# Queries and keys split ahead of their transposes, and a second score pass on exchanged query halves

## What is computed

```python
B, H, S, D = 4, 8, 576, 64
scores = matmul(q, k.T) / 8.0
s_pos = maximum(s, 0.0); cum = cumsum(s_pos, -1)
bias = -(cum[:, :, :, None] - cum[:, :, None, :])
scores = where(causal, -1e9, scores + minimum(bias, 0.0))
attn = exp(scores - max(scores)); attn = attn / (sum(attn) + 1e-09)
x = matmul(attn, v)                       # 32 heads of 576 x 64
# then: layer norm + relu MLP (512 -> 2048 -> 512), a rank-32 mix over tokens, a second MLP
```

## Time and profile before

| | |
|---|---|
| time, median of 3 runs (lowest, highest) | 1116.39 us (1112.28, 1117.29) |
| the profiled execution | 1115.07 us, its span 1113.3 us |
| granted TensorE clock, mean | 0.992 |
| busy share of the span | TensorE 94%, its weight load 84%, VectorE 73%, ScalarE 50%, GpSimd 31% |
| instructions | 21040 |
| DMA | 118.71 MB in 156260 packets, mean 107 GB/s |

### The profile page before, as it was taken

The page is one execution under the profiler, slowest core; times in us unless marked ns, Lnnn a source line. Parts: engine busy times, 40 slices in busy tenths (PEclk is TensorE's granted clock), DMA queues, the critical chain, the costliest instruction groups (busy, mean ns, idle before and its releaser), DMA issues.

```text
span 1113.3 us, 21040 instructions
## 1 busy us (share of the span) xinstructions
PE 1051.2 (94%) x6936; PEld 931.8 (84%) x6936; DVE 811.7 (73%) x1732; ACT 557.2 (50%) x1265; POOL 339.6 (31%) x377
## 2 busy tenths in 40 slices
PE   6788888888797999999999999999999999999998
PEld 5677777777687898889888889888889888888887
DVE  6899999999558768767767757976865866765532
ACT  5788888888444344444444434443423432433321
POOL 1154453211116433333324232333232423332100
PEclk9999999999898999999999999999999999999999
DMA  5745545445241321322231343432142133223131
GB/s 155 233 120 132 126 120 130 127 119 159 83 134 64 108 76 57 123 68 77 76 114 58 114 151 107 156 112 82 62 138 96 66 100 121 75 84 114 58 127 44
DMA packets 156260, 118.71 MB, mean 107 GB/s; under 512 B 86496, under 2 KB 131552, under 8 KB 156192
## 3 DMA queue, kind: packets, MB, share of 16 engines
q1 hardware_dynamic: 156192, 117.80, 35.2%
HBM read 98.82 MB, written 18.95 MB: 106 GB/s over the span
## 4 chain that ended last, share of the span: by engine, by line
PE 89%; DVE 3%; ACT 3%; issue 2%; DMA 1%; SPq 1%; POOL 0%; ACTq 0%; DVEq 0%; POOLq 0%
PE ps_up L751 9%; PE ps_up L752 9%; PE ps_up L753 9%; PE ps_acc L798 6%; PE ps_acc L797 6%; PE ps_acc L799 6%; PE ps_s L798 5%; PE ps_s L797 5%; PE ps_s L799 5%; PE ps_x L681 5%; PE ps_s L651 3%; PE ps_pt L662 3%; ACT prob L928 2%; PE ps_up L662 2%; PE ps_up L627 2%
## 5 line engine op out<-in xcount | busy, mean ns | idle before, releaser
L751 PE MATMUL ps_up<-z,w 128*128 128x256 f32 x896 | 255.6, 285 | 4.7 <-DVE z L1270 3.8
L752 PE MATMUL ps_up<-z,w 128*128 128x256 f32 x896 | 254.4, 284 | 0.0
L753 PE MATMUL ps_up<-z,w 128*128 128x256 f32 x896 | 254.4, 284 | 0.0
L564 POOL TENSOR_TENSOR w_f<-raw 128x256 f32<-128x256 f32 x64 | 69.0, 1078 | 412.1 <-DMA raw<-in_moe_w_ch 397.4
L751 PEld LDWEIGHTS ps_up<-z,w 128*128 128x128 f32 x896 | 172.3, 192 | 10.6 <-DVE z L1270 4.2
L752 PEld LDWEIGHTS ps_up<-z,w 128*128 128x128 f32 x896 | 172.5, 193 | 5.1
L753 PEld LDWEIGHTS ps_up<-z,w 128*128 128x128 f32 x896 | 172.8, 193 | 0.0
L797 PE MATMUL ps_acc<-w_hi,h 128*128 128x512 f32 x320 | 126.7, 396 | 1.9 <-DVE x_res L1296 1.9
L798 PE MATMUL ps_acc<-w_lo,h 128*128 128x512 f32 x320 | 126.8, 396 | 0.0
L799 PE MATMUL ps_acc<-w_hi,h 128*128 128x512 f32 x320 | 126.2, 394 | 0.0
L1093 ACT ACTIVATE h<-cs 128x768 fp32r<-128x768 f32 x64 | 54.1, 846 | 126.8 <-DVE cs L1383 126.8
(11 more groups left out here) (170 smaller groups left out, 2642.7 us busy)
## 6 DMA issues: line engine op xcount, KB each, us to landing
raw<-in_moe_w_ch SPq DMA_DIRECT2D x80, 512.0 KB, 3.6
ncum_b<-ncum_dram SPq DMA_DIRECT2D x32, 288.0 KB, 3.5
x_in<-x_dram SPq DMA_DIRECT2D x18, 512.0 KB, 4.3
k_raw<-in_k SPq DMA_DIRECT2D x64, 128.0 KB, 2.5
u_dram<-x_in SPq DMA_DIRECT2D x9, 512.0 KB, 2.8
q_raw<-in_q SPq DMA_DIRECT2D x32, 128.0 KB, 3.2
v_raw<-in_v SPq DMA_DIRECT2D x32, 128.0 KB, 2.2
w_f<-in_moe_w_ch SPq DMA_DIRECT2D x4, 1024.0 KB, 8.1
```

Source lines behind the costliest of these rows:

```text
L564: pool.tensor_tensor(to[:, I5, 1], a21, a22, ALU.add).then_inc(s1_done, 1)
L751: nc.tensor.matmul(bank, w_hi, z_hi, start=(start and c == 0), stop=False, skip_group_check=True)
L752: nc.tensor.matmul(bank, w_hi, z_lo, start=False, stop=False, skip_group_check=True)
L753: last = nc.tensor.matmul(bank, w_lo, z_hi, start=False, stop=(stop and c == 1), skip_group_check=True)
```

## The change

- Queries, keys and their last tile are no longer split after the transposes but before. GpSimd makes the high and low part of the raw rows side by side (`split_rows`: `split_queries`, `split_keys`, `split_last`, two instructions each), for head u+2 ahead of `split_values(u)`. TensorE then transposes 128-column tiles that hold both, so that high parts come out in partitions 0 to 63 and low parts in 64 to 127.
- ScalarE copies the queries out of PSUM with one instruction (`copy_q`, where `q_high` was), VectorE the keys (`copy_k`, where `k_low` was) and the last tile of both (`copy_last`). `q_low`, `k_high` and `last_high` are gone.
- The two score passes use the same keys (hi over lo). The first has the queries as they are (hi with hi, lo with lo), the second has the query halves exchanged, in `q_swap`. The exchange is made by DMA inside SBUF, two transfers of 64 partitions for the 512 columns and two for the last 64: `swap_queries`, `swap_last`.
- Keys are loaded once, in the row order of the queries; the last tiles are loaded once. `load_last` runs one head further ahead.
- SP's list has a new order. Buffers of raw rows are free when GpSimd has split them, not when TensorE has transposed them.
- The slices of w2 are split in halves (high or low part), spread over heads 2 to 29.
- TensorE's score tile 0 waits for the exchanged queries too, tile 4 for the exchanged last tile.

```diff
             def load_q(u):
-                wait(sp, qt_done, u)
+                wait(sp, q_lo_done, u)
                 sp.dma_start(q_raw[:], flat_rows(q_f, u)).then_inc(q_loaded, 16)
             def load_k(u):
-                wait(sp, kt_done, u)
-                for a in range(2):
-                    sp.dma_start(k_raw[:, :, a], whole_tiles(k_f, u)).then_inc(k_loaded, 16)
+                wait(sp, k_lo_done, u)
+                sp.dma_start(k_raw[:], flat_rows(k_f, u)).then_inc(k_loaded, 16)
             def load_last(u):
-                waits_apart(sp, (lt_done, u))
+                waits_apart(sp, (l_lo_done, u))
                 for flat, to in ((q_f, slice(0, LAST)), (k_f, slice(LAST, P))):
-                    sp.dma_start(last_raw[to], last_tile(flat, u).unsqueeze(1).to_broadcast([LAST, 2, D])).then_inc(last_loaded, 16)
+                    sp.dma_start(last_raw[to, 0], last_tile(flat, u)).then_inc(last_loaded, 16)
+            def swap_queries(u, p):
+                waits_apart(sp, (q_done, u + 1))
+                for to, of in ((slice(0, D), slice(D, P)), (slice(D, P), slice(0, D))):
+                    sp.dma_start(q_swap[p][to, 0:FULL].bitcast(F32), qk[p][of, 0, 0:FULL].bitcast(F32)).then_inc(q_swapped[p], 16)
+            def swap_last(u, p):
+                waits_apart(sp, (l_done, u + 1))
+                for to, of in ((slice(0, D), slice(D, P)), (slice(D, P), slice(0, D))):
+                    sp.dma_start(q_swap[p][to, FULL:S].bitcast(F32), qk[p][of, 0, FULL:S].bitcast(F32)).then_inc(l_swapped[p], 16)
             def head_alone(m, p, first=False):
                 u = 2 * m + p
+                if exists(u + 3):
+                    load_q(u + 3)
+                    load_k(u + 3)
+                if exists(u + 1):
+                    swap_last(u + 1, 1 - p)
+                if exists(u + 3):
+                    load_last(u + 3)
                 if exists(u + 2):
-                    load_last(u + 2)
+                    load_sums(u + 2, p)
+                    swap_queries(u + 2, p)
                 if exists(u + 1):
                     load_v(u + 1)
-                if exists(u + 2):
-                    load_sums(u + 2, p)
-                if exists(u + 3):
-                    load_q(u + 3)
                 if not first:
                     store_head(*before(m, p))
-                if exists(u + 3):
-                    load_k(u + 3)
...
             load_last(1)
             load_q(2)
             load_k(2)
+            for p in range(2):
+                swap_queries(p, p)
+            swap_last(0, 0)
+            load_last(2)
...
+            def split_rows(u, x, split, loaded, transposed, hi_done, lo_done):
+                pool.wait_ge(*loaded)
+                waits_apart(pool, (transposed, u))
+                pool.tensor_tensor(split[:, :, 0, :], x[:], one[:].unsqueeze(2).to_broadcast(x.shape), ALU.mult).then_inc(hi_done, 1)
+                pool.wait_ge(hi_done, u + 1)
+                pool.tensor_tensor(split[:, :, 1, :], x[:], split[:, :, 0, :].bitcast(F32), ALU.subtract).then_inc(lo_done, 1)
...
+            split_queries(0)
+            split_keys(0)
+            split_last(0)
+            split_queries(1)
+            split_keys(1)
+            split_last(1)
             pool.wait_ge(pads_done, 1)
             for u in range(HEADS):
+                if u + 2 < HEADS:
+                    split_queries(u + 2)
+                    split_keys(u + 2)
+                    split_last(u + 2)
                 split_values(u)
-                if 4 <= u < 4 + JC:
-                    split_second(u - 4)
+                for half in range(halves(u), halves(u + 1)):
+                    split_second(half // 2, half % 2)
...
+            def transpose_rows(bank, split):
+                to = bank.rearrange("d (n t) -> d t n", t=QT - 1)
+                for t in range(QT - 1):
+                    last = nc.tensor.transpose(to[:, t], twice(split[:, t]).bitcast(F32), ident)
+                return last
...
             def scores(m, p, i):
                 u = 2 * m + p
-                q2, k_hi, k_lo = (a[p] for a in (q2s, k_his, k_los))
                 if i == 0:
-                    pe.wait_ge(q_lo_done, u + 1)
-                    pe.wait_ge(k_lo_done, u + 1)
-                    pe.wait_ge(l_lo_done, u + 1)
+                    pe.wait_ge(q_done, u + 1)
+                    pe.wait_ge(k_done, u + 1)
+                    pe.wait_ge(l_done, u + 1)
+                    pe.wait_ge(q_swapped[p], 32 * (m + 1))
+                if i == QT - 1:
+                    pe.wait_ge(l_swapped[p], 32 * (m + 1))
...
-                    for n, kk in enumerate((k_hi, k_lo)):
-                        last = nc.tensor.matmul(bank, q2[:, i * P:(i + 1) * P], kk[:, lo:hi], start=(n == 0), stop=(n == 1 and not diag))
+                    for n, qq in enumerate((qk[p][:, 0], q_swap[p][:])):
+                        last = nc.tensor.matmul(bank, qq[:, i * P:(i + 1) * P], qk[p][:, 1, lo:hi], start=(n == 0), stop=(n == 1 and not diag))
...
+            def copy_q(m, p):
                 act.wait_ge(qt_done, 2 * m + p + 1)
+                nc.scalar.activation(qk[p][:, 0, 0:FULL], up[0][:, 0:FULL], ACT.Copy, scale=-SCALE).then_inc(q_done, 1)
...
+            def copy_k(m, p):
+                dve.wait_ge(kt_done, 2 * m + p + 1)
+                nc.vector.tensor_copy(qk[p][:, 1, 0:FULL], k_bank(2 * m + p)[:, 0:FULL]).then_inc(k_done, 1)
+            def copy_last(m, p):
+                dve.wait_ge(lt_done, 2 * m + p + 1)
+                nc.vector.tensor_tensor(qk[p][:, :, FULL:S], up[0][:, 0:P].rearrange("p (a n) -> p a n", a=2),
+                                        last_scale[:].unsqueeze(2).to_broadcast([P, 2, LAST]), ALU.mult).then_inc(l_done, 1)
```

More of the change, by code:

```diff
@@ L161, in chain_kernel @@
             prob_2_0 = sbuf("prob_2_0", [P, FULL], F32, small)
-            q2s = [sbuf(f"q2{p}", [P, SP_PAD], F32R, small) for p in range(2)]
+            q_swap = [sbuf(f"q_swap{p}", [P, SP_PAD], F32R, small) for p in range(2)]
             prob_3 = sbuf("prob_3", [P, FULL], F32, small)
@@ L234, in chain_kernel @@
         l_hi_done, l_lo_done = sem("l_hi_done"), sem("l_lo_done")
+        q_done, k_done, l_done = sem("q_done"), sem("k_done"), sem("l_done")
+        q_swapped, l_swapped = [sem(f"q_swapped{p}") for p in range(2)], [sem(f"l_swapped{p}") for p in range(2)]
         v_hi_done, v_split = sem("v_hi_done"), sem("v_split")
@@ L615, in transpose_q @@
-                for t in range(QT - 1):
-                    last = nc.tensor.transpose(bank[:, t], q_raw[:, t], ident)
-                last.then_inc(qt_done, 1)
+                waits_apart(pe, (q_lo_done, u + 1), (l_done, u))
+                transpose_rows(up[0], q_split).then_inc(qt_done, 1)
             def transpose_k(m, p):
                 u = 2 * m + p
-                pe.wait_ge(k_loaded, 32 * u + 32)
+                pe.wait_ge(k_lo_done, u + 1)
                 if not (isinstance(u, int) and u == 0):
-                    pe.wait_ge(q_lo_done, u + 1)
@@ L625, in transpose_k @@
[L625 to L628, removed]
+                    pe.wait_ge(q_done, u + 1)
+                transpose_rows(k_bank(u), k_split).then_inc(kt_done, 1)
             def transpose_last(m, p):
                 u = 2 * m + p
-                pe.wait_ge(last_loaded, 32 * u + 32)
-                pe.wait_ge(k_lo_done, u + 1)
@@ L635, in transpose_last @@
-                nc.tensor.transpose(up[0][:, 0:P], twice(last_raw[:]), ident).then_inc(lt_done, 1)
+                pe.wait_ge(l_lo_done, u + 1)
+                pe.wait_ge(k_done, u + 1)
+                if isinstance(u, int) and u == 0:
+                    pe.wait_ge(q_done, u + 1)
+                nc.tensor.transpose(up[0][:, 0:P], twice(last_split[:, 0]).bitcast(F32), ident).then_inc(lt_done, 1)
             def scores(m, p, i):
                 u = 2 * m + p
-                q2, k_hi, k_lo = (a[p] for a in (q2s, k_his, k_los))
@@ L948, in head_alone @@
                 probs_high(m, p, 1)
-                if not final:
-                    last_high(*after(m, p))
                 exponential(m, p, 3)
@@ L955, in head_alone @@
                 if more:
-                    q_high(*second(m, p))
+                    copy_q(*second(m, p))
                 if final:
@@ L966, in head_alone @@
                 probs_high(m, p, 4)
-                if more:
-                    k_high(*second(m, p))
                 if not final:
@@ L1064, in prepare @@
                     second_high(j)
-            q_high(0, 0)
-            k_high(0, 0)
-            last_high(0, 0)
+            copy_q(0, 0)
             exponential(0, 0, 0)
-            q_high(0, 1)
+            copy_q(0, 1)
             exponential(0, 0, 1)
-            k_high(0, 1)
             attention(act, head_alone)
@@ L1201, in head_alone @@
                     weights_low(0)
-                if more:
-                    q_low(*second(m, p))
                 if not final:
```

(2 more changed lines are left out.)

76 lines of the change are left out of this document (32 added, 44 removed).

## The result

The changed kernel takes 1140.14 us (median of 4 runs, 1138.43 to 1141.77); the kernel before, run beside it, 1115.73 us (1112.28 to 1117.29). The ratio is 1.020, 95% interval 1.017 to 1.023: about 24 us slower, clearly more than nothing. The direction that was held likeliest is right, the size is not, and 1140 lies above the range of 1113 to 1138.

What follows compares the result with a forecast made beforehand. Bound: a loop of TensorE's queue and ScalarE's tile-3 copy and tile-4 exponential, 8.28 us a head. Sum: 1115.1 + 5.0 (start) - 1.5 (w2 loads) + 1.7 (TensorE) + 4 (SP's queue) = 1124.3, say 1124 us; range 1113 to 1138.

Steps and rivals of the forecast that it cites:

- What bounds a head: Attention stage: a loop of TensorE's queue (6.75 us) and ScalarE (1.53 us), 8.28 us, without VectorE.
- Rival D: Attention heads: the freed VectorE and ScalarE shorten the head, TensorE's wait goes at most whole; 1089 us, chance 0.08.
- SP's queue: SP's issuing of transfers in the looped heads: a little over the loop's period, +4 us.
- 6.7 + 4s: SP's time per head in us after the change, with four swaps at s each; 8.66 us forecast.
- s: Price of issuing one swap on SP: taken as 0.49 us, between 0.34 and 0.66.
- Rival C: SP's queue: swaps as dear to issue as the doubled last tile, 0.66 us; 1142 us, chance 0.10.
- The lead of 3 us: Looped heads: some 3 us that SP can fall behind before its lateness costs time.
- The start: First heads: splits and swaps queued behind load_k(2) delay the first score to 14.6 us; +5.0 us, bounds +4.3 and +6.4.
- The w2 loads: Early heads: TensorE's waits for last-tile loads behind 2 MB of weights go; -1.5 us, bounds -2.6 and 0.
- TensorE, +1.7: Query transposes in the loop, as wide as the keys': 287 ns each, not 273; +1.7 us for 30 heads.
- Rival E: Key transposes, written to PSUM with a stride of four columns, slow down; 1137 us, chance 0.05.
- GpSimd: Splits of raw rows on GpSimd: 0.58 + 0.69 us for 256 columns, 6.9 of 8.33 us a head; costs 0 in steady state.

Runs made afterwards that it cites:

- x1: The changed kernel without its four swap transfers per head and the waits on them, cross products of high and low parts left out; 1112.32 us, ratio 0.996.
- x5: x1 with the exponential of tile 4 issued on ScalarE ahead of copy_q and the tile-3 copy; 1099.96 us, ratio 0.985.
- x2: The kernel before with four unread transfers inside SBUF, of 64 partitions each, added per looped head on SP; 1172.27 us, ratio 1.050.
- x10: The kernel before with two unread transfers inside SBUF, of 128 partitions each, added per looped head on SP; 1139.77 us, ratio 1.019.
- x3: The changed kernel with the first query swap and first last-tile swap moved earlier in SP's list; 1135.76 us, ratio 1.017.
- x6: The changed kernel, complete, with the two loads of v per head issued by ScalarE and not by SP; 1125.12 us, ratio 1.007.
- x8: The changed kernel without the two last-tile swaps per head, cross products of that tile left out; 1119.61 us, ratio 1.002.
- x11: The kernel before with two unread transfers of 128 partitions from DRAM into SBUF added per looped head on SP; 1129.83 us, ratio 1.012.

## Why the prediction was off

**What bounds a head: right.** The loop of TensorE and ScalarE, with no VectorE in it, was read from the earlier trace rows. x1 takes 0.7 to 1.0 us a head off both engines and keeps the 8.28 us. Rival D is out. It has a condition that I had not seen: with ScalarE's order changed the same relief gives 12 us (x5).

**SP's queue: the right mechanism, the wrong size, and this is the step that failed.** The formula 6.7 + 4s holds: with the 0.57 us measured it gives 8.98, and SP took 9.01. I took s = 0.49, the row of a 64-row load from DRAM, because it had the same number of partitions, and wrote that the price was in no row. For these transfers within SBUF partitions hardly set it (x2 and x10: 0.59 and 0.56), and the same transfer costs less out of DRAM (0.56 against 0.42). A nearer row stood in the trace of before, and I had overlooked it: the store of a head's last 64 rows, which has the same number of partitions and its source in SBUF.

```profile
101.35 0.58 SPq L385 DMA_DIRECT2D x_dram<-x_head  x1
```

SBUF as the source is not the whole price either: the store of the other 512 rows, out of 128 partitions, takes 0.42. The choice between 0.49 and the doubled tile's 0.66 decided over some 18 us. At 0.57, and with TensorE's period as it was measured, my reckoning gives 26 x (8.98 - 8.34) - 3 = 13.6 us for the loop, where I had put 4 and 1.7; 15.5 were lost. The term is steep: 0.01 us of s is worth 1 us of time. With such a slope a point value and half of C in the range were too little.

This step is the largest part of the miss and not all of it. The profiled execution, 1141.8 us, lies 17.5 above the forecast of 1124.3: 9.8 in the loop, 4.4 at the w2 loads, 1.5 in the last head, 1.3 in the rest of the span, 0.5 at the start. With s at 0.57 and the other terms as forecast the sum would have been 1132, still inside the range. Rival C, with a chance of 0.10, decides from 0.55 on, so the case is C's; that its 1142 lies so near the 1140 measured is luck, for it stands for s = 0.66.

**The lead of 3 us: not shown.** After the stalls of the w2 loads, TensorE next stands as long as this for a swap at 89.74, four heads later, when SP at the measured pace had lost 4 x 0.67 = 2.7 us:

```profile
89.74 0.32 PE L711 MATMUL ps_s<-qk 128*128 128x128 f32 x1 [1.05 <-DMA q_swap<-qk]
```

That fits a lead of about 3 us, but how far ahead SP was after those stalls no row tells, so it is not shown.

**The start: right.** The first score was put at 14.6 us, the total at +5.0 (+4.3 to +6.4); 15.05 and +5.5 were measured. The mechanism is the one named, the swaps behind `load_k(2)`: they were issued at 12.01, and x3, which moves them, gets 3.9 us back.

```profile
15.05 0.45 PE L711 MATMUL ps_s<-qk 128*128 128x128 f32 x1 [5.35 <-DMA q_swap<-qk]
```

**The w2 loads: wrong in sign.** I let both waits for raw rows go and kept 1 us for `swap_last(3)`. They did go, but two swaps of the last tile wait in their place, the first of which I had not reckoned:

```profile
40.87 0.40 PE L711 MATMUL ps_acc<-qk 128*128 128x288 f32 x1 [1.15 <-DMA q_swap<-qk]
...
52.04 0.41 PE L711 MATMUL ps_acc<-qk 128*128 128x288 f32 x1 [2.61 <-DMA q_swap<-qk]
```

3.76 us against 2.58. A load has its slack of a head or more; a swap is made between a copy and its use and has little, so it is the worse thing to queue behind 2 MB. The other 1.6 us of this stretch is the second head, 9.84 us long against 8.27, which runs while the clock is below full (0.85 as a mean from 20 to 30 us). It is not the swaps' doing: x1 has none, and its second head takes 9.83 us (clock 0.83 as a mean from 20 to 30 us).

**TensorE, +1.7: 0.** The query transposes stayed at 273 ns, although twice the partitions go in. The difference to the keys in the earlier trace rows was not one of width; what it is no run shows. **Rival E** is refuted: 286 ns with the stride.

**GpSimd: right.** Its splits, with those of the kernel after from 100 to 250 us beside VectorE's copy of the keys:

```profile
L579 POOL TENSOR_TENSOR q_split<-q_raw,q_split 128x256 fp32r<-128x256 f32 x17 | 12.4, 731 | 1.3
...
L1164 DVE CAST qk<-ps_up 128x512 fp32r<-128x512 f32 x17 | 11.7, 686 | 0.0
...
L577 POOL TENSOR_TENSOR q_split<-q_raw,one 128x256 fp32r<-128x256 f32 x17 | 10.4, 612 | 0.0
```

0.61 + 0.73 against the predicted 0.58 + 0.69, and nobody waits for GpSimd in the loop.

**What I had not reckoned with: the clock.** TensorE's wait of 1.05 us at 89.74 costs more than itself. Behind it, after only 1.4 us of work, comes the wait for the exponential that every head has:

```profile
92.22 0.77 PE L722 MATMUL ps_pt<-ident_f,prob 64*128 64x64 f32 x5 [1.08 <-ACT prob L979]
```

By itself this second wait doesn't lower the clock: before, it comes in every head while the granted clock is 1.00. Here the clock falls just ahead of 92 us. The windows (stretch, length, busy time and instructions of TensorE, its weight load, VectorE, ScalarE and GpSimd, granted clock, DMA share, GB/s):

```profile
90.00:92.00 2.00, 1.14 (x12) 0.83 (x11) 0.94 (x4) 1.27 (x4) 1.64 (x3) 0.95 0.46 140
92.00:94.00 2.00, 1.78 (x10) 1.69 (x11) 0.94 (x3) 0.90 (x4) 1.92 (x3) 0.50 0.12 24
94.00:96.00 2.00, 2.00 (x11) 1.60 (x9) 1.18 (x4) 0.60 (x2) 1.62 (x3) 0.50 0.78 193
96.00:98.00 2.00, 2.00 (x11) 1.48 (x10) 1.26 (x5) 1.26 (x4) 0.00 (x0) 0.50 0.84 206
...
100.00:103.00 3.00, 2.30 (x23) 1.99 (x21) 1.80 (x7) 2.53 (x5) 2.45 (x3) 1.00 0.28 78
```

For 6 us the granted clock is 0.50, that is 1.2 GHz. The head that holds the swap wait takes 9.59 us, the one behind it, over half of it at half the clock, 11.16. From 60 to 260 us the mean granted clock is 0.97 after the change, 0.96 in x10, 0.88 in x2, and 1.00 before and in x1, x6 and x8. In the loop I read it as a symptom more than a cause: while TensorE is slow SP gains on it, the next heads run at 8.28 to 8.58 again, and the mean is back near SP's pace (8.91 and 9.01). SP's own rounds show no trace of it: from 62 us on, up to the last but one, each takes between 8.87 and 9.15 us. At the end, where SP has nothing left to catch up, it costs its full price: the last head is 1.5 us longer and runs at 0.50 from 300 to 303 us. No run changes the clock alone, so this reading is argued and not shown. Why the last head is slow in some kernels (after, x1, x2, x11) and not in others (before, x3, x8) stays open. So do the 1.3 us in the rest of the span, which are about as large as the spread of the runs.

## What to carry to other kernels

An engine that only issues transfers has a length of its own per round: take the time it waits off its round, add the new issues, and compare with the round of the bounding loop before looking at bytes or landing times. Where that comparison is close, a guessed issue price is not good enough: go through all issues of the queue, the stores too, for the row nearest in source, destination and partitions, and give the range the whole span between the rows. And when an engine is relieved beside the loop that bounds, ask what order of work would bring the relief into the loop; here that order was worth nothing without the change, and 12 us with it.

## What the runs showed of the hardware

- Issuing a transfer within SBUF from SP takes 0.55 to 0.59 us, for 64 or 128 partitions and for 64 or 512 columns (after, x2, x10), and 0.42 us for the same transfer from DRAM (x11). The store of a head from SBUF to DRAM takes 0.42 us for 128 partitions and 0.58 for 64 (before, medians over all heads).
- A swap half of 128 KB lands 3.7 us (median) after its issue in the kernel after, the query load of 128 KB in the same kernel 2.1. It is not the halving alone: in x2 halves of 128 KB within SBUF, issued back to back, land after 2.3 us, and in x10 the same bytes in one transfer of 256 KB after 2.4. In the kernel after the swap stands right behind the load of the sums (288 KB, 3.9 us to landing); whether that is the cause no run shows. The Trainium skill (DMA: Bandwidth & Descriptors, Rules for kernel authors), by which two transfers to disjoint halves serialize, is neither borne out nor refuted by this; no run here moved one half alone.
- VectorE copies 128x512 float32 out of PSUM in 686 ns, as long as the subtraction of that shape took before (`k_low`, L1125, 686 ns): turning the one into the other saved nothing on VectorE.
- Two waits of TensorE of about 1 us, 1.4 us of work apart, were followed by some 6 us at half the granted clock (after, 88.69 to 98 us). One such wait in each head was not (before, 1.08 us a head at a clock of 1.00).
